# First block's convolution with undivided taps, its feature exchange on ScalarE, three tiles begun together, and the last 64-row store issued from ScalarE

## The reference

```python
w = softmax(weight, axis=-1)                  # 8 heads x 7 taps: exp(w - max) / (sum + 1e-9)
y[b, s, c] = sum_k w[head(c), k] * x_pad[b, s + k, c]   # causal, 6 zeros ahead; 2 x 4096 tokens, 192 features
g = sigmoid(y @ w_gate) * (y @ w_val)         # 192 -> 1536
y = g @ w_out                                 # 1536 -> 192
h = y @ w_in                                  # 192 -> 2048
out = where(h > 0, h, exp(min(h, 0)) - 1) @ w_out2      # 2048 -> 192
```

## Time and profile before

| | us |
|---|---|
| median of 3 runs (1221.04 to 1221.27) | 1221.19 |
| the profiled execution | 1220.55 |
| its span, first to last instruction | 1218.7 |
| PE busy | 1199.1 (98%) |
| DVE busy | 920.6 (76%) |
| ACT busy | 625.0 (51%) |
| POOL busy | 83.9 (7%) |

### The profile page before, as it was taken

How to read it: one execution, slowest core, us unless ns; L and a number is a source line. 1 busy time by engine, 2 the same in 40 slices (tenths; PEclk the granted TensorE clock), 3 DMA queues, 4 the chain that set the end, 5 groups by cost and what they waited for, 6 DMA issues and landing times.

```text
span 1218.7 us, 27112 instructions
## 1 busy us (share of the span) xinstructions
PE 1199.1 (98%) x10220; PEld 970.4 (80%) x10220; DVE 920.6 (76%) x1503; ACT 625.0 (51%) x1083; POOL 83.9 (7%) x84
## 2 busy tenths in 40 slices
PE   5999999999999999999999999999999999999998
PEld 3988888888888888888888888888888888888886
DVE  7787777777777877778777777777777777787786
ACT  4545545455454645545455454554535545455554
POOL 3541001010010100101000010100101001010000
PEclk9999999999999999999999999999999999999999
DMA  6311101001010010100101001110101101001000
GB/s 201 90 36 37 31 18 34 25 22 30 17 34 30 17 30 17 34 30 17 30 17 47 17 17 30 35 30 17 24 23 35 30 17 34 30 17 30 12 8 26
DMA packets 14342, 39.09 MB, mean 32 GB/s; under 512 B 2288, under 2 KB 2288, under 8 KB 14320
## 3 DMA queue, kind: packets, MB, share of 16 engines
q1 hardware_dynamic: 14176, 38.78, 11.3%
q10 hardware_dynamic: 144, 0.01, 0.0%
HBM read 15.71 MB, written 6.29 MB: 18 GB/s over the span
## 4 chain that ended last, share of the span: by engine, by line
PE 97%; DVE 2%; DMA 1%; ACT 0%; issue 0%; SPq 0%; DVEq 0%; ACTq 0%
PE hid L219 54%; PE z_acc_a L257 9%; PE y_acc_a L257 7%; PE z_acc_b L257 6%; PE z_acc_a L269 5%; PE y_acc_b L257 5%; PE y_acc_a L269 4%; PE z_acc_b L269 3%; PE y_acc_b L269 2%; DVE mixed L578 1%; DVE hidden L637 0%; DMA ys<-ys 0%; DMA cw<-conv_w 0%; PE y_acc_a L280 0%; PE y_acc_b L280 0%
## 5 line engine op out<-in xcount | busy, mean ns | idle before, releaser
L219 PE MATMUL hid<-xs,gw 64*128 64x512 f32 x3240 | 619.4, 392 | 0.0
L219 PEld LDWEIGHTS hid<-xs,gw 64*128 64x128 f32 x3240 | 486.3, 184 | 71.6
L219 PE MATMUL hid<-ys,ew 64*128 64x512 f32 x2160 | 475.4, 392 | 0.0
L440 ACT CAST h_split<-hidden 128x512 fp32r<-128x512 f32 x448 | 276.6, 618 | 313.4 <-DVE hidden L637 273.1
L219 PEld LDWEIGHTS hid<-ys,ew 64*128 64x128 f32 x2160 | 362.9, 184 | 49.3
L435 ACT ACTIVATE curve<-hid 128x512 f32<-128x512 f32 x448 | 265.6, 597 | 260.8 <-PE hid L219 260.8
L600 DVE TENSOR_TENSOR h_split<-hidden,h_split 128x512 fp32r<-128x512 f32 x448 | 314.6, 702 | 36.6 <-ACT h_split L440 31.4
L637 DVE TENSOR_TENSOR hidden<-hid,curve 128x512 f32<-128x512 f32 x192 | 132.8, 691 | 152.9 <-PE hid L219 128.2
L257 PE MATMUL z_acc_a<-h_split,ew 64*128 64x512 f32 x720 | 187.0, 392 | 0.0
L269 PE MATMUL z_acc_a<-h_split,ew 64*128 64x512 f32 x720 | 187.0, 392 | 0.0
L669 DVE SCALAR_TENSOR_TENSOR hidden<-hid,below 128x512 f32<-128x512 f32 x256 | 177.1, 692 | 8.8
(11 more groups left out here) (82 smaller groups left out, 943.4 us busy)
## 6 DMA issues: line engine op xcount, KB each, us to landing
x_in<-x_windows SPq DMA_DIRECT2D x16, 518.0 KB, 3.2
ys<-ys SPq DMA_DIRECT2D x32, 256.0 KB, 3.6
xs<-xs SPq DMA_DIRECT2D x32, 256.0 KB, 3.7
out<-z_out SPq DMA_DIRECT2D x16, 256.0 KB, 2.0
raw_g<-g_weights SPq DMA_DIRECT2D x12, 288.0 KB, 4.0
raw_e<-e_weights SPq DMA_DIRECT2D x8, 384.0 KB, 4.8
out<-z_out SPq DMA_DIRECT2D x16, 128.0 KB, 2.3
x_in<-x_windows SPq DMA_DIRECT2D x2, 259.0 KB, 2.8
```

Source lines behind the costliest of these rows:

```text
L219: return nc.tensor.matmul(acc[:], w[rows, at:at + P], inp[rows, features], start=s == 0, stop=s == HID - 1)
L440: nc.scalar.copy(h_split[:, t % RING, 0], hidden[:, t % RING]).then_inc(hi_done, 1)
```

## The change

It has these parts.

1. The first block is mixed with the taps before they are divided: `raised = exp(w - max)` comes from ACT with the bias `cw_neg`, and the division by the sum is a factor `cw_inv` in ACT's hi part and DVE's lo part (`split_first`). The sum, its increment and its reciprocal lie between DVE's taps. Tap 0 of each group is a multiplication on ACT. POOL writes the divided `taps` for the other blocks.
2. The exchange of the first block's features (`ys[:, 4:6]`) is four half-width ACT operations instead of two DMAs.
3. `opening` begins tiles 0, 1 and 2; tile 2 has the two `y_acc` banks, which block one does not use otherwise. Steps 3 to 11 follow; tile 11 is in the `y_acc` banks again. Shares come four tiles behind (`LAG = 4`), so step 3 has 9 pairs, and block two's first two steps take two shares each, 19 pairs instead of 19 and 14.
4. Weights: six raw buffers for g tiles, g0 loaded ahead of x, `AHEAD = 4`, and the last 64 columns' lo part is four tiles behind the rest on POOL, which begins after 13 taps. On SP, x of block two and e0 to e3 come ahead of g6 to g11.
5. Block two's taps are at t = 3 to 9 of block one and its features are split at t = 10, before `hidden`. Block three's taps are two tiles later too.
6. ACT issues the last block's 64-row store; SP issues only the 128-row one.

```diff
-RAW_SLOTS = 4
-AHEAD = 3
-BY_DVE = 2
+RAW_G_SLOTS = 6
+RAW_E_SLOTS = 4
+AHEAD = 4
+LAG = 4
...
+        def gate_val(n_is_first, t):
+            if n_is_first and t in (2, NG - 1):
+                return y_acc
+            at = 2 * ((t + 1) % 2 if n_is_first and t > 2 else t % 2)
+            return hid[at:at + 2]
...
 (SP)
+            load_g(0)
             sp.dma_start(x_in[:, 0], x_windows[0][:, 0]).then_inc(x_first, 16)
             sp.dma_start(x_in[:, 1], x_windows[0][:, 1]).then_inc(x_loaded, 16)
-            for t in range(RAW_SLOTS):
+            for t in range(1, RAW_G_SLOTS):
                 load_g(t)
-            swap_x(0, ys)
-            load_g(RAW_SLOTS)
-            for p in range(RAW_SLOTS):
-                load_e(p)
             sp.wait_ge(tap_done, 2 * K)
             load_x(1)
-            for t in range(RAW_SLOTS + 1, NG):
+            for p in range(RAW_E_SLOTS):
+                load_e(p)
+            for t in range(RAW_G_SLOTS, NG):
                 load_g(t)
             swap_x(1)
...
-            store_b(BLOCKS - 1)
             store_a(BLOCKS - 1)
...
 (PE, opening)
+                pe.wait_ge(x_hi, 1)
+                for t in range(3):
+                    pe.wait_ge(g_hi, t + 1)
+                    both(t, 0, 0)
+                wait_g_lo(pe, 0)
+                both(0, 0, 2)
+                pe.wait_ge(x_ready, 1)
+                for t in range(3):
+                    both(t, 0, 1)
+                pe.wait_ge(x_exchanged, 2)
+                for t in range(3):
+                    both(t, 1, 0)
+                both(0, 1, 2)
+                pe.wait_ge(x_exchanged, 4)
+                for t in range(3):
+                    both(t, 1, 1)
+                pe.wait_ge(x_hi, 2)
+                both(0, 2, 0)
+                both(0, 2, 2)
+                both(1, 2, 0)
+                both(2, 2, 0)
+                pe.wait_ge(x_ready, 2)
+                for t in range(3):
+                    both(t, 2, 1)
+                for t in range(1, 3):
+                    wait_g_lo(pe, t)
+                    for part in range(3):
+                        both(t, part, 2)
...
 (PE, g_phase)
+                for t in range(0 if prev else 3, NG):
+                        shares = [g_tile_share(t - LAG, base, acc)] if t >= LAG else []
+                        shares = [g_tile_share(NG - LAG + 2 * t + h, base - NG, z_acc) for h in range(2)]
+                    elif t < 2 or (prev is None and t in (3, 4)):
+                        pe.wait_ge(hidden_done, base - 2 + t)
+                    else:
+                        pe.wait_ge(hidden_done, base + t - 1)
...
 (ACT)
             set_table(ACT.Exp, 0)
+            split_g_weights(0)
+            act.wait_ge(cw_maxed, 1)
+            for c in range(2):
+                nc.scalar.activation(raised[:, c], cw[:, c], ACT.Exp, bias=cw_neg[:, c:c + 1]).then_inc(cw_exped, 1)
+            act.wait_ge(x_first, 16)
+            nc.scalar.mul(mixed[:, 0], x_in[:, 0, 0:T], raised[:, 0, 0:1]).then_inc(tap_done, 1)
+            act.wait_ge(x_loaded, 16)
+            nc.scalar.mul(mixed[:, 1], x_in[:, 1, 0:T], raised[:, 1, 0:1]).then_inc(first_tap, 1)
+            split_g_weights(1)
+            split_g_weights(2)
+            set_table(ACT.Sigmoid, 1)
+            act.wait_ge(cw_step, 3)
+            act.wait_ge(tap_done, K)
+            nc.scalar.mul(ys[:, 0], mixed[:, 0], cw_inv[:, 0:1]).then_inc(x_hi, 1)
+            nc.scalar.mul(ys[UP, 4], mixed[LOW, 0], cw_inv[LOW, 0:1]).then_inc(x_exchanged, 1)
+            nc.scalar.mul(ys[LOW, 4], mixed[UP, 0], cw_inv[UP, 0:1]).then_inc(x_exchanged, 1)
+            act.wait_ge(x_ready, 1)
+            nc.scalar.copy(ys[UP, 5], ys[LOW, 1].bitcast(F32)).then_inc(x_exchanged, 1)
+            nc.scalar.copy(ys[LOW, 5], ys[UP, 1].bitcast(F32)).then_inc(x_exchanged, 1)
+            split_g_weights(3)
+            act.wait_ge(tap_done, 2 * K)
+            nc.scalar.mul(ys[:, 2], mixed[:, 1], cw_inv[:, 1:2]).then_inc(x_hi, 1)
...
+            act.wait_ge(z_b_done, BLOCKS)
+            act.dma_start(out[P:OUT, T * (BLOCKS - 1):T * BLOCKS], z_out[LOW, 1]).then_inc(stored, 16)
...
 (DVE, g_phase)
+                    if prev is None and t == NG - 2:
+                        split_x(1, 0, xs)
+                        split_x(1, 1, xs)
...
-                    m = 2 * (t - (3 if prev else 2))
+                    m = 2 * (t - (5 if prev == "G" else 3))
...
 (DVE, start)
+            nc.vector.tensor_reduce(cw_neg[:], cw[:], AX_X, ALU.max, negate=True).then_inc(cw_maxed, 1)
             first_lo(0)
+            raised_tap(1)
+            nc.vector.tensor_reduce(cw_sum[:], raised[:], AX_X, ALU.add).then_inc(cw_step, 1)
+            raised_tap(2)
+            nc.vector.tensor_scalar(cw_den[:], cw_sum[:], 1e-9, None, ALU.add).then_inc(cw_step, 1)
+            raised_tap(3)
+            nc.vector.reciprocal(cw_inv[:], cw_den[:]).then_inc(cw_step, 1)
+            for m in range(4, K):
+                raised_tap(m)
+            raised_tap(K + 1)
+            split_first(0)
+            for m in range(K + 2, 2 * K):
+                raised_tap(m)
+            first_lo(1)
+            split_first(1)
...
 (POOL)
+            pool.wait_ge(tap_done, 2 * K - 1)
+            for t in range(2, LAG):
+                split_g_weights(t)
+            for t in range(LAG, NG):
+                split_g_last_columns(t - LAG)
+                split_g_weights(t)
```

More of the change, by code:

```diff
@@ L98, in ffn_kernel @@
         x_loaded = sem("x_loaded")
-        g_loaded = [sem(f"g_loaded{i}") for i in range(RAW_SLOTS)]
-        e_loaded = [sem(f"e_loaded{i}") for i in range(RAW_SLOTS)]
+        g_loaded = [sem(f"g_loaded{i}") for i in range(RAW_G_SLOTS)]
+        e_loaded = [sem(f"e_loaded{i}") for i in range(RAW_E_SLOTS)]
         g_hi = sem("g_hi")
@@ L192, in _ @@
             load_x(2)
-            for p in range(RAW_SLOTS, PAIRS):
+            for p in range(RAW_E_SLOTS, PAIRS):
                 load_e(p)
@@ L212, in _, with hid_mm @@
         def _(pe):
-            def hid_mm(rows, acc, w, inp, s):
+            def hid_mm(rows, acc, w, inp, s, last=HID - 1):
                 part, kind = divmod(s, 3)
@@ L219, in hid_mm @@
                 return nc.tensor.matmul(acc[:], w[rows, at:at + P], inp[rows, features],
-                                        start=s == 0, stop=s == HID - 1)
+                                        start=s == 0, stop=s == last)
             def g_tile_share(t, base, acc):
@@ L253, in share_mm @@
                     if begins == "a":
-                        wait(pe, low_a_done, step - 3)
+                        wait(pe, low_a_done, step - LAG)
                     if begins == "b":
@@ L297, in opening, with both @@
[L297 to L300, removed]
-                both(0, 2)
-                pe.wait_ge(x_swapped, 32)
-                both(0, 3)
-                both(0, 4)
-                both(0, 5)
-                both(1, 3)
-                both(1, 4)
-                wait_g_split(pe, 1)
-                both(1, 2)
-                both(1, 5)
-                pe.wait_ge(x_ready, 2)
-                for t in range(2):
-                    for s in range(6, HID):
-                        both(t, s)
+                def both(t, part, kind):
+                    s = 3 * part + kind
+                    last = 7 if t == 0 else 8
+                    gate, val = gate_val(True, t)
+                    lower = hid_mm(LOW, gate, gw[:, t], inp, s, last)
+                    upper = hid_mm(UP, val, gw[:, t], inp, s, last)
+                    if s == last:
+                        lower.then_inc(hid_done, 1)
+                        upper.then_inc(val_done, 1)
@@ L328, in g_phase @@
                     elif prev == "G":
-                        before = [[9, 10], [11]][t]
-                        shares = [g_tile_share(h, base - NG, z_acc) for h in before]
+                        shares = [g_tile_share(NG - LAG + 2 * t + h, base - NG, z_acc) for h in range(2)]
                     else:
@@ L485, in g_phase @@
                         split_g_weights(t + AHEAD)
-                    if prev is None and t == NG - 3:
-                        split_x(1, 0)
-                        split_x(1, 1)
                     hi_part(base, t)
```

177 lines of the change are left out of this document (88 added, 89 removed).

## The result

The changed kernel takes 1227.95 us (median of 6 runs, 1226.36 to 1229.5), the kernel before 1221.27 (6 runs, 1221.04 to 1221.41): ratio 1.0057, 95% interval 1.0044 to 1.0070. It is 6.7 us slower; 1220.1 was forecast, 1222.8 was the end of the range. The profiled execution took 1228.0 us with a span of 1225.9 (before: 1220.55 and 1218.7).

What follows compares the result with a forecast made beforehand. PE was taken as the bound, with 97% of the chain and 15.0 us idle in the first block. Gains 0.6 + 0.45 = 1.05 us took the profiled run from 1220.55 to 1219.5, median 1220.1; range 1217.0 to 1222.8.

Steps and rivals of the forecast that it cites:

- The loops between are not touched.: Between start and end of the kernel: the change is worth only what it takes off those two.
- Start of block two, 52.4: Block two starts at 52.4 to 53.3 us after an exchange wait of 3 us or more; lead 0.6 us at 52.4.
- My own upper pace of 3.18: DVE's seven tiles before block two's split: 3.05 to 3.18 us each.
- The lead of 4.8 us at step 3: End of the opening: step 3 starts at 19.9 us (19.2 to 20.4) against 24.71, a lead of 4.8 us.
- the hidden exchange: First block: ACT's exchange copies end near 12.7 us and hide behind PE, removing the 2.42 us wait.
- 15.6 to 16.3: Opening, second feature group: DVE's last tap ends at 15.6 to 16.3 us, later if beside POOL.
- g6: Weight tile 6, loaded behind x and e0 to e3: lands between 24.0 and 26.0 us, 24.0 taken, delaying `hidden` of tile 3.
- my own sign that this loss is wrong: No ACT wait on DMA ahead of the cast of g6, and no PE wait on `hidden` ahead of step 5.
- The stall of 1.2 us: PE ahead of step 5 waits 1.2 us (0.5 to 3.2) for `hidden` of tile 3, free at 26.5 us.
- The clock: Slower rival, chance 0.22: the exchange wait drops PE to 1.2 GHz from 3.1 us idle, giving 1221.5 to 1222.8 us.
- Block three's taps: Taps moved to t = 5 to 11, where DVE waited for PE before: nothing, up to 0.5 us each way.
- The end: Last two stores both issued at 1215.3 us: a gain of 0.45 us (0.1 to 0.55).

Runs made afterwards that it cites:

- e0: Not a run: a weight tile of the kernel, whose load on SP the change puts ahead of g6 to g11; no time of its own.
- e2: The kernel before with only block three's taps moved later, to t = 5 instead of t = 3: 1220.15 us.
- e8: The kernel before with one unused tensor of 56 bytes per partition ahead of `taps`, no instruction changed: 1225.81 us.
- e9: The kernel before with `raw_g` two unused slots (4608 bytes) larger, no instruction changed: 1221.24 us.
- e4: The changed kernel with block two's taps a step earlier, at t = 2 to 8, and its split at t = 9 behind `hidden`: 1225.11 us.
- e5: The changed kernel with POOL's wait ahead of its first weight subtraction on the second half of the split features instead of on 13 taps: 1228.4 us.
- e16: e13 with 32 unused bytes ahead of `taps` and g6 loaded ahead of weight tiles e0 to e3: 1219.42 us.
- e7: The changed kernel with `raised` and the two added `raw_g` slots moved behind `z_out`, restoring the later tensors' old addresses: 1222.45 us.
- e19: e7 with 32 unused bytes ahead of `taps`: 1219.65 us.
- e18: e13 with xs and ys alone moved to a multiple of 128 bytes by two unused tensors: 1214.32 us.
- e13: The changed kernel with the edits of e7, e4, e5 and e3 together: 1219.51 us.
- e1: The changed kernel with block three's taps put back to t = 3: 1228.76 us.
- e3: The changed kernel with PE's waits for `hi_done` and `low_a_done` put ahead of the step's first matmul: 1227.53 us.
- e10: The kernel before with 32 unused bytes ahead of `taps`, so xs, ys, hidden and h_split begin at a multiple of 128: 1216.48 us.
- e17: The kernel before with 32 unused bytes ahead of `taps`, block three's taps at t = 5 and the last 64-row store issued by ACT: 1214.89 us.

## Why the prediction was wrong

By its own steps, against the profiled run (1219.5 forecast, 1228.0 measured, 8.5 us off):

- **"The loops between are not touched."** This failed, and it is the largest term, which the sum had at nothing: 4.35 us as the remainder above, 4.8 by e2, 4.6 by e8. No instruction of the loops changed, but their operands' address did; e8 and e9 show it without any other difference.
- **Start of block two, 52.4.** 55.34 came, 2.9 us late; the mechanism was right (a wait of 3.31 us after DVE's chain, where "3 us or more" was forecast; e4 removes it), the sizes were not. `hidden` of tile 3 began at 27.07 instead of 25.8, and the seven tiles to the first split took 49.92 - 27.07 = 22.85 us, 3.26 each, instead of 3.05. My own upper pace of 3.18 was too low. DVE was busy for 22.79 of the 22.85 us. POOL worked 15.7 us beside it, against 13.3 in the 22.87 us from 25.86 before, so it met more of DVE's operations and not fewer, as I had assumed for 3.05; that this alone made the difference was not tried. The last 0.2 us are the first split of the features (0.81 for 0.68) and the way from its end to block two (4.61 for 4.53). The second split took longer still, but the exchange was issued at 50.76 and 51.34 without waiting for it:

```profile
27.07 0.68 DVE L687 TENSOR_TENSOR hidden<-hid,curve 128x512 f32<-128x512 f32 x1
49.92 2.51 DVE L633 TENSOR_TENSOR xs<-mixed,xs 128x512 fp32r<-128x512 f32 x2
```

- **The lead of 4.8 us at step 3** was 3.3: step 3 began near 21.4 (step 4's first share at 23.55, less 9 pairs). The start (11.16 for 11.0) and the hidden exchange were right. "15.6 to 16.3" for the last tap held (it ended at 15.77), and so did the hi part (16.52). What failed is the lo part behind them, to which I gave no time: DVE's subtraction of weights and the second `split_first` came after the last tap, 1.4 us without POOL (e5) and 3.5 beside it. I had counted POOL against one tap only.
- **g6.** It landed at 19.39 + 5.1 = 24.5, as forecast, but ACT was not idle for it: its cast at 24.54 shows no DMA wait, which was my own sign that this loss is wrong. PE's 0.80 us ahead of step 5 ended with `hidden` of tile 3, which followed a lo part of 1.07 us beside POOL. The stall of 1.2 us was right in size only by two thirds, and for another reason. The wait for g6 was only hidden by the late opening: with the earlier one of e5 it came, 0.54 us.
- **The clock.** The forecast left it to a rival with a chance of 0.22, deciding from 3.1 us of idleness. The wait was 3.31, and it fell: 1.5 us, where I had 1.4. The condition itself was wrong, for no length of wait divides the cases. Of the eleven waits of 1.8 to 3.4 us on PE behind the opening in the changed kernel's programs, nine were followed by starts 0.43 us apart (1.88 in e4, 2.53 in e16, 2.66 in e7, 2.70 in e19, 2.79 in e18, 2.89 in e13, 3.24 in e1, 3.31, and 3.33 in e5) and two were not (1.83 in e16, 3.19 in e3). It should have been the likelier case.
- **Block three's taps:** -0.47 by the wait, within "0.5 each way"; -0.9 by e2, beyond it. **The end:** -0.47 for -0.45.

Off by 4.35 + 2.9 + 1.5 - 0.47 - 0.02 = 8.26; the remaining 0.24 lie outside the span (2.1 us around it for 1.85). Without the pace the median would have been near 1227.95 - 4.35 = 1223.6 by this sum, outside the range that ends at 1222.8; e7, with the old addresses, took 1222.45, just inside. Its block two began 1.0 us earlier than the changed kernel's (54.35), and why is open. Either way the other misses had used up the range by themselves, and the address carried the time far out of it.

## What to carry to other kernels

When a change adds a tensor or resizes a buffer, compare the matmul count of a long undisturbed window before looking at the edited part; if it differs, put the allocation back at the old remainder by 128 bytes, and try the streamed operands at 0. Time won at the start is worth only what the longest chain behind it leaves: follow that chain (here 14 taps on DVE) to the next point where all engines meet. A wait of 2 to 3 us on TensorE should carry the price of its restart (here about 1.5 us) in the sum, not in a rival. And a start taken from one profiled run can be 0.8 us off by itself; look at the same moment in a second run of the same order of work.

## What the hardware did that was not expected

- A matmul pair of 512 columns takes 0.2342, 0.2338, 0.2332 or 0.2323 us in programs that differ in the operands' addresses, with clock 1.00 and no wait in any row. The Trainium skill ("SBUF — State Buffer", Who interferes with whom) says that only the pair of ports of DVE and GpSimd causes contention, and that TensorE shares its read ports with nobody; what else makes a read slower at some starts is open. The cause is shown as far as the address, not in its mechanism.
- The same program with all operands at 0 has two times 4.7 us apart (e10: 1216.4 and 1221.09; e17: 1214.9 and 1219.63).
- The granted clock doesn't always fall together with the wait. It fell during a wait of 3.33 us in e5 (0.79 over it), and in e7 and e13 it still read 0.99 and 0.98 for 1.4 us behind waits of 2.66 and 2.89 us and then 0.50.
- An ACT multiplication by a per-partition pointer took 0.72 us where the cast of that size takes 0.62, in the changed kernel's trace; the sum had left this out:

```profile
15.80 0.72 ACT L581 ACTIVATE ys<-mixed,cw_inv 128x512 fp32r<-128x512 f32 x1 [1.23 <-DVE mixed L619]
```
